# One core, attention into two mixer MLPs: the last two attention heads and the first MLP weights are placed anew

## The reference

```python
# attention: q, k, v are [2, 8, 768, 64]: 16 heads of 768 tokens
q_bucket, k_bucket = hash bits of q @ proj, k @ proj
scores = 64 ** -0.5 * (q @ k.T), -1e9 where q_bucket != k_bucket
attn = exp(scores - rowmax) / (rowsum + 1e-9);  x = attn @ v          # -> [2, 768, 512]
# first MLP
u = x + real(fft over tokens and features of x)
x = u + relu(layernorm(u) @ w_ch1) @ w_ch2
# second MLP
h = gelu(x @ w_in); a, v = h[..., :512], h[..., 512:]
x = x + (a * (w_sg @ (layernorm(v) * g_ln) + b_sg)) @ w_out
```

## Time and profile before

| | |
|---|---|
| median of 3 runs | 727.71 us (727.67 to 727.96) |
| the profiled execution | 727.84 us, of which the span of instructions is 726.0 us |
| PE busy | 713.9 us (98%) |
| DVE busy | 480.6 us (66%) |
| ACT busy | 382.2 us (53%) |
| POOL busy | 347.7 us (48%) |
| chain that ended last | PE 88%, DVE 7%, all else under 2% each |
| granted TensorE clock | full in all 40 slices |

### The profile page before, as it was taken

The page is one execution under the profiler, slowest core; times in us unless marked ns, Lnnn a source line. Parts: engine busy times, 40 slices in busy tenths (PEclk is TensorE's granted clock), DMA queues, the critical chain, the costliest instruction groups (busy, mean ns, idle before and its releaser), DMA issues.

```text
span 726.0 us, 11758 instructions
## 1 busy us (share of the span) xinstructions
PE 713.9 (98%) x3905; PEld 589.8 (81%) x3905; DVE 480.6 (66%) x701; ACT 382.2 (53%) x708; POOL 347.7 (48%) x341
## 2 busy tenths in 40 slices
PE   9999999999999999999999999999999999999998
PEld 8856666666675899988888888999998888888886
DVE  6877778787876799885655578544434675347533
ACT  4777888788876535554444554445442454125300
POOL 4178878887887920044633142546642355005400
PEclk9999999999999999999999999999999999999999
DMA  4332323232323150032211211822003000010001
GB/s 96 69 77 62 83 56 76 61 81 55 76 65 109 54 175 1 1 97 78 58 59 59 59 58 33 287 81 65 30 1 145 1 1 1 29 59 1 0 15 73
DMA packets 71076, 45.20 MB, mean 62 GB/s; under 512 B 44996, under 2 KB 61560, under 8 KB 70520
## 3 DMA queue, kind: packets, MB, share of 16 engines
q1 hardware_dynamic: 70456, 41.19, 20.7%
q0 software_dynamic: 576, 3.43, 1.3%
HBM read 35.42 MB, written 3.15 MB: 53 GB/s over the span
## 4 chain that ended last, share of the span: by engine, by line
PE 88%; DVE 7%; issue 1%; ACT 1%; POOL 1%; DMA 1%; SPq 0%; POOLq 0%; ACTq 0%; DVEq 0%
PE PS L814 83%; DVE un L2018 2%; DVE mneg L1780 1%; PE PS L838 1%; PE PS L1101 1%; PE PS L1318 1%; PE PS L1272 1%; DMA ops<-mrow 1%; PE PS L1263 1%; PE PS L953 1%; DVE st L2006 0%; DVE W1L L2051 0%; DVE ops L1751 0%; DVE ops L1772 0%; DVE ops L1745 0%
## 5 line engine op out<-in xcount | busy, mean ns | idle before, releaser
L814 PE MATMUL PS<-ops 98*128 98x384 f32 (+1 forms) x576 | 134.8, 359 | 3.4 <-DMA ops<-mrow 1.1
L814 PEld LDWEIGHTS PS<-ops 98*128 98x128 f32 (+1 forms) x576 | 95.4, 190 | 44.1 <-ACT E L1387 19.6
L1780 DVE TENSOR_REDUCE mneg<-PS 128x1 f32<-128x768 f32 x96 | 91.5, 956 | 36.9 <-PE PS L814 36.2
L1387 ACT ACTIVATE E<-PS 128x384 f32<-128x384 f32 x192 | 83.5, 487 | 44.7 <-PE PS L814 43.9
L664 POOL TENSOR_TENSOR esum<-esum,E 128x768 f32<-128x768 f32 x56 | 102.5, 1830 | 2.8 <-ACT E L1387 0.3
L649 POOL TENSOR_TENSOR W2L<-W2R,W2H 128x1024 fp32r<-128x1024 f32 x16 | 38.8, 2426 | 111.8 <-ACT W2H L1371 111.8
L2067 DVE SCALAR_TENSOR_TENSOR hL<-pre,hH 128x384 fp32r<-128x384 f32 x42 | 43.8, 1043 | 51.1 <-ACT hH L1632 51.1
L814 PE MATMUL PS<-BH,W1H 128*128 128x384 f32 x228 | 76.9, 337 | 0.4 <-DVE hL L2067 0.2
L814 PE MATMUL PS<-BH,W1L 128*128 128x384 f32 x228 | 76.9, 337 | 0.0
L814 PE MATMUL PS<-BL,W1H 128*128 128x384 f32 x228 | 76.2, 334 | 0.0
L814 PE MATMUL PS<-W2H,hH 128*128 128x512 f32 x192 | 75.5, 393 | 0.0
(11 more groups left out here) (211 smaller groups left out, 1595.1 us busy)
## 6 DMA issues: line engine op xcount, KB each, us to landing
W1R<-in_moe_w_ch_dram SPq DMA_DIRECT2D x32, 256.0 KB, 3.1
W2R<-in_moe_w_ch_dram SPq DMA_DIRECT2D x32, 256.0 KB, 2.9
ops<-ops SPq DMA_DIRECT2D x30, 192.0 KB, 3.0
qk<-in_k_dram SPq DMA_DIRECT2D x32, 96.0 KB, 2.4
qk<-in_q_dram SPq DMA_DIRECT2D x32, 96.0 KB, 2.4
vn<-in_v_dram SPq DMA_DIRECT2D x32, 96.0 KB, 2.4
out_dram<-X SPq DMA_DIRECT2D x12, 256.0 KB, 2.0
WsgR<-in_moe_w_sg_dram SPq DMA_DIRECT2D x1, 2304.0 KB, 8.1
```

The costliest lines, as they stand in the source:

```text
L814: return pe.matmul(dst, lhs, rhs, start=start, stop=stop, **kw)
L1387: act.activation(A["E"][:, e_slot(t, 0, kt), half(a)], PS[:, ST_BANK + a, 0:HALF], ACT.Exp, scale=EXP_SCALE).then_inc(exp_done, 1)
L1780: dve.tensor_reduce(A["mneg"][:, s, j:j + 1], PS[:, bank:bank + 2, 0:HALF], AX.XY, ALU.max, negate=True).then_inc(max_done, 1)
```

## The change

- `late` now holds for head 15 alone; head 14 takes the ordinary form. So POOL gets five `sum_exponentials` for it at time 14, ACT `raw_output` and `raw_sums` at time 15, PE `denominators` and `turn_back`, SP `place_sums`. The separate output bank of head 15 is given up.
- PE's time 15 is written out as `last_head`: scores and values of head 15 alternate by key tile, with head 14's last values and `denominators` ahead of `scores(2)`, and its `turn_back` ahead of `scores(4)`. Head 15's last values, once at time 16, are part of it.
- ACT: `weights_hi(0)` and `w2_upper(0)` leave time 14 and come behind `fold_hi` of passes 2 and 3.
- POOL: `weight_sums(1)` moves from time 14 to time 15; `first_weights_lower` and `w2_lower(0)` come behind the attention, each ahead of a `reciprocal_deviation` of the layer norm; T1L is loaded at time 14, between the fourth and the fifth sum; T2H and T2L are loaded at the end of time 15.
- DVE: `fold_lo(0)` goes ahead of head 14's `head_output`.

```diff
         def late(t, ahead):
-            return not t.looped and t.head(ahead) >= HEADS - 2
+            return not t.looped and t.head(ahead) >= HEADS - 1
...
@@ POOL
-                if not t.looped and t.head(0) == HEADS - 1:
-                    pool.wait_ge(rows_in, 32 * (HEADS - 1))
-                    load_first_table(A["T1L"], t1_lo)
-                    load_second_tables()
...
                 if t.has(1):
                     matches(t, 1)
+                if not t.looped and t.head(0) == HEADS - 2:
+                    pool.wait_ge(rows_in, 32 * (HEADS - 1))
+                    load_first_table(A["T1L"], t1_lo)
                 if t.has(0) and not late(t, 0):
                     sum_exponentials(t, 0, 4)
-                if not t.looped and t.head(0) == HEADS - 2:
+                if is_last(t):
                     weight_sums(1)
-                    first_weights_lower()
-                    w2_lower(0)
                 if t.has(-1):
                     finish_head(t, -1)
+                if is_last(t):
+                    load_second_tables()
...
-            for block in range(2):
-                reciprocal_deviation(0, block)
+            first_weights_lower()
+            reciprocal_deviation(0, 0)
+            w2_lower(0)
+            reciprocal_deviation(0, 1)
@@ PE
+            def last_values(t, kt):
+                g, s = t.head(0), t.slot(0)
+                if kt == 0:
+                    pe.wait_ge(v_in[s], 32 * t.turn(0) + 32)
+                    pe.wait_ge(mean_done, g + MEAN_FREE)
+                    pe.wait_ge(vsum_step, g + 1)
+                    mm(PS[:, PV_BANK, MEAN_AT:MEAN_AT + D], ones[:, :], A["vsum"][:, s, :], True, True)
+                pe.wait_ge(exp_done, 2 * T * g + 2 * kt + 2 + EXP_FREE)
+                for j in range(T):
+                    last = mm(PS[:, PV_BANK, j * (D + 1):(j + 1) * (D + 1)], A["E"][:, e_slot(t, 0, kt), tile(j)],
+                              A["vn"][:, s, kt, :], False, kt == T - 1, skip_group_check=True)
+                if kt % 2:
+                    last.then_inc(pv_step, 1)
+
+            def last_head(t):
+                scores(t, 0, 0)
+                scores(t, 0, 1)
+                values(t, -1, 2)
+                denominators(t, -1)
+                scores(t, 0, 2)
+                last_values(t, 0)
+                scores(t, 0, 3)
+                last_values(t, 1)
+                turn_back(t, -1)
+                scores(t, 0, 4)
+                last_values(t, 2)
+                scores(t, 0, 5)
+                for kt in range(TH, T):
+                    last_values(t, kt)
@@ ACT
                 if t.has(-1) and not late(t, -1):
                     raw_output(t, -1)
+                if is_last(t):
+                    raw_sums(t, -1)
...
-                if t.has(-1) and not late(t, -1):
+                if t.has(-1) and not late(t, -1) and not is_last(t):
                     raw_sums(t, -1)
...
-                if not t.looped and t.head(0) == HEADS - 2:
-                    weights_hi(0)
...
-                if not t.looped and t.head(0) == HEADS - 2:
-                    w2_upper(0)
...
                 if b + 1 < B:
                     fold_hi(2 * b + 2)
                     fold_hi(2 * b + 3)
+                    weights_hi(0)
+                    w2_upper(0)
@@ DVE
+                if pass1:
+                    fold_lo(0)
                 if t.has(-1):
                     head_output(t)
                 if pass1:
-                    fold_lo(0)
                     fold_features(1, 0)
```

More of the change, by code:

```diff
@@ L261, in late, with is_last @@
         def late(t, ahead):
-            return not t.looped and t.head(ahead) >= HEADS - 2
-        def out_bank(t, ahead):
-            return SUM_BANK if late(t, ahead) and t.head(ahead) == HEADS - 1 else PV_BANK
+            return not t.looped and t.head(ahead) >= HEADS - 1
+        def is_last(t):
+            return not t.looped and t.head(0) == HEADS - 1
         def e_sum(t, ahead):
@@ L918, in values @@
             def values(t, ahead, part):
-                g, s, bank = t.head(ahead), t.slot(ahead), out_bank(t, ahead)
+                g, s, bank = t.head(ahead), t.slot(ahead), PV_BANK
                 if part == 0:
                     pe.wait_ge(v_in[s], 32 * t.turn(ahead) + 32)
[L922 to L925, removed]
+                    pe.wait_ge(mean_done, g + MEAN_FREE)
                     pe.wait_ge(vsum_step, g + 1)
@@ L929, in values @@
                 for kt in (2 * part, 2 * part + 1):
[L930 to L937, removed]
-                last.then_inc(pv_step, 1)
+                    for a in range(2):
+                        last = mm(PS[a * D:(a + 1) * D, bank, 0:HALF], A["vn"][:, s, kt, 0:D],
+                                  A["E"][:, e_slot(t, ahead, kt), half(a)], kt == 0, kt == T - 1)
+                last.then_inc(pv_step, 1)
+            def last_values(t, kt):
+                g, s = t.head(0), t.slot(0)
+                if kt == 0:
+                    pe.wait_ge(v_in[s], 32 * t.turn(0) + 32)
+                    pe.wait_ge(mean_done, g + MEAN_FREE)
+                    pe.wait_ge(vsum_step, g + 1)
[21 more added lines that the diff above has]
+                    last_values(t, kt)
             def denominators(t, ahead):
@@ L1049, in one_time @@
                 t = Time(it, u)
+                if is_last(t):
+                    last_head(t)
+                    return
                 if t.has(0):
@@ L1057, in one_time @@
                     scores(t, 0, 1)
-                if t.has(-1):
+                if t.has(-1) and not late(t, -1):
                     values(t, -1, 2)
@@ L1795, in value_mean @@
                 dve.wait_ge(x_done, g - 1 + X_FREE)
-                dve.tensor_scalar(A["vmean"][:, t.slot(-1, 2), :], PS[:, out_bank(t, -1), MEAN_AT:MEAN_AT + D], 1.0 / S, None,
+                dve.tensor_scalar(A["vmean"][:, t.slot(-1, 2), :], PS[:, PV_BANK, MEAN_AT:MEAN_AT + D], 1.0 / S, None,
                                   ALU.mult).then_inc(mean_done, 1)
@@ L1803, in head_output @@
                     dve.wait_ge(pv_step, PV_PARTS * g + PV_PARTS)
-                    bank, at = out_bank(t, -1), MEAN_AT + D
+                    bank, at = PV_BANK, MEAN_AT + D
                     raw = PS[:, bank, 0:T * (D + 1)].rearrange("p (j w) -> p j w", j=T)
```

## The result

| | before | after |
|---|---|---|
| median | 727.73 us (727.67 to 727.96) | 740.82 us (740.58 to 741.41) |
| profiled execution | 727.84 us, span 726.0 | 740.58 us, span 738.7 |
| granted TensorE clock, mean over the span | full | 0.982 |

The ratio is 1.0182 (interval 1.0169 to 1.0196): 13.1 us slower, where 3.0 were forecast. The sign and the place were right, the size was four times too small.

The account below looks back on a forecast made before the run. PE was taken as the bound, with DVE nearly full in the first transform. 727.84 (profiled run) + 2.7 (attention) + 0.3 (moved weights) = 730.84, median 0.13 lower: 730.7 us; own range 729.3 to 731.9, range with rivals 726.8 to 733.2.

Parts of the forecast that it names:

- What bounds the kernel: Whole span: PE busy for 98%; in the first transform, 263.0 to 282.0, DVE is nearly full too, 17.63 of 19.0 us.
- What PE saves: Head 14's three parts of values in ordinary form save 3.6 us, denominators and turn_back add 1.25: net 2.4 us less.
- the first limit: scores(15, 0) waits for head 15's row maxima, placed by SP: starts at 244.0, gain 1.4 us, wait 1.0 us.
- The second limit: denominators(14) waits for POOL's fifth sum, which takes turns with DVE's folds: PE waits 2.9 us, bounds 0 to 2.9.
- the bound of 249.9: On POOL at time 14: the fifth sum's end if POOL wins the first turn, against 250.4 as walked.
- rival C: DVE's fold_tokens(1) gets ahead of the fifth sum: PE waits 4.7 us, total 732.5 us; chance 0.12.
- PE and DVE from there: After denominators(14): head 15's values end at 263.4, second_transform(0) gets DVE's result at 275.35; term +2.7 us, bounds -1.8 and +4.5.
- The forecast without the clock: Whole kernel: the walk's total with no clock fall counted, 730.7 us.
- the term for the moved weights: After the attention: W1's lower halves and w2_lower(0) on POOL meet DVE's work; +0.3 us, bounds 0 and 1.2.
- rival D: PE's waits of 1.0 and 2.9 us cost its clock: 4.5 us of work at half speed add about 2.3, 733.0 us; chance 0.08.
- Rival A: POOL at 239 to 247.5: turns are loose, PE's saving comes through, -1.8 us, 725.9 us; chance 0.14.

Follow-up runs that it names:

- alt_early_output: Kernel before with head 15's scores and values alternating, and on DVE its mean and output read ahead of two folds: 728.06 us, ratio 1.0003.
- alt_weights: Kernel before with the weights moved as in the change and head 15 alternating, head 14 still in late form: 729.03 us, ratio 1.0018.
- short_sums: Changed kernel with sums 2 to 5 of head 14 on POOL cut to 8 of 768 columns: 728.51 us, ratio 0.9998.
- fill: Changed kernel with nine float32 identity matmuls, results never read, put on PE ahead of denominators(14): 732.44 us, ratio 1.0059.
- wide_short: Changed kernel with 12 matmuls of 384 columns, results never read, behind scores(15, 2): 734.0 us, ratio 1.0088.
- fill_both: Changed kernel with nine identity matmuls ahead of denominators(14) and eight more ahead of second_transform(0): 731.47, 734.46, 739.59 and 742.12 us, ratio 1.0102.
- weights_only: Kernel before with only the weights moved as in the change, heads 14 and 15 late and in old order: 728.84 us, ratio 1.0008.
- stall_attention: Kernel before with one added PE wait for a tiny DMA ahead of values(14, 2): 741.6, 742.9 and 744.5 us, ratio 1.0216.
- wide_after_fall: Changed kernel with 24 matmuls of 384 columns, results never read, behind scores(15, 2): 735.0 us, ratio 1.0096.
- stall_mlp: Kernel before with the added PE wait for a tiny DMA in the first MLP, step 6: four runs 729.54 to 729.86, two 733.0 and 733.3 us; ratio 1.0039.

## Why the prediction was wrong

**What bounds the kernel: right.** PE first, DVE nearly full from 263 us on. Three kernels that ended the attention 1.5 to 3.2 us earlier (alt_early_output, alt_weights, short_sums) all met DVE there.

**What PE saves, and the first limit: right.** 1.44 us per part, `scores(15, 0)` 1.3 us earlier in the profile (with the earlier start of that trace taken off), where 1.4 were walked, and a wait of 0.92 where 1.0 was walked.

**The second limit: right in mechanism and nearly in size.** The wait was 2.27 us where 2.9 were walked. The second sum won the first turn (issued at 238.67, Z at 238.69), which the walk had as the bound of 249.9; one of the two small POOL operations came between Y and Y, the other ran beside the last Y, and the fifth sum ended at 250.0 on the time scale of the trace before, instead of 250.4. The order of fifth sum and `fold_tokens(1)` was the walked one, so rival C did not come. What the turns did not give is the fold's length of 4.00 us, with its end at 252.3. It should have had its turn after the fifth sum, at 249.7; instead POOL's next operation, which began 1.4 us after the fold and ran its usual 1.00 us from 249.67, went ahead of it too, in fill and wide_short as well. What the Trainium skill says of the shared port (SBUF — State Buffer, "Who interferes with whom"), that the engine which issues second waits for the whole instruction, fits the fold and the fifth sum, issued 0.4 us earlier; it does not fit this next operation.

**PE and DVE from there: right at full clock, in part by luck.** The transform starts at 263.5 in fill (263.35 in its own trace), walked 263.4. But two errors cancel in this: the first matmul of head 15's values comes at 252.8 instead of 252.2, since the fold was held longer, and from there PE needs 10.7 us instead of 11.2. PE's wait for DVE is 2.2 us, walked 2.15. The forecast without the clock was 730.7; the runs of this order at full clock took 731.40 (fill) and 731.47 (fill_both). Of the missing 0.7 us, 0.3 to 0.4 are in the term for the moved weights (0.3 taken, 0.6 to 0.7 in wide_short and weights_only), and 0.2 in the start of `second_transform(0)` (275.6 on the scale of before, walked 275.35).

**The clock: this is the step that failed.** The forecast's sum has no term for it; it stood in rival D with 0.08 and +2.3 us. Two things in it were mis-sized. *The price*: I took the length of a fall from the start of the kernel, 4.5 us. There PE does `keep_clock` matmuls and wide ones; behind the wait of this change it does late-form values of 65 columns. Measured: 27.3 us low. From the first matmul of head 15's values to the transform PE takes 20.16 us (252.53 to 272.69) where fill takes 10.67, so 9.5 more, and to the end of the first transform 12.0 more; 2.2 of this is taken back, as the wait for DVE vanishes beside a slower PE. That leaves 9.8 at `second_transform(0)` (285.06 against 275.42, each from its own start of the values), and 9.4 between the times, 740.82 less 731.40 at full clock. *The chance*: the fall came in four of four runs of the change, and with an added wait of 1.75 us in the three runs of stall_attention (means of 0.977 to 0.982 in both). I had argued that no wait of the trace before was long enough to show it, and made this a reason for a small chance; it was a reason for a wide one. With the measured 9.4 in place of 2.3 the forecast's 730.7 becomes 740.1; that is a check of the sum, and no derivation of the price.

The Trainium skill's rule, that an idle array is put to half its clock until it has been busy again (TensorE: Matmul & The Clock Gate, "What's actually happening"), pointed at the right mechanism. The runs show more than it: in the change, stall_attention and the low run of fill_both, PE was busy without a break in the windows from 256 to 268 and stayed at half speed; the clock came back at 278.3, 279.0 and 277.6, 4 to 7 us after the first matmuls of 194 columns. With matmuls of 384 columns right behind the wait it fell for a few microseconds at most (wide_short, wide_after_fall), and with 384 and 512 columns it fell briefly or not at all (stall_mlp).

**Rival A** (the saving comes through) would have failed even with loose turns: short_sums had no collision at all and came out level with before. `second_transform(0)` starts 1.0 us earlier there and not 1.8 (271.72 in its own trace, against 272.82), the moved weights take some 0.7 back, and a fall of 3.4 us behind PE's wait for DVE takes up to 1.7 (half of it) more. The bound left out the last.

Left open: which of column count, number format and share of time spent loading weights makes the clock stay low under the late-form matmuls. They differ from the wide ones in all three, and no run separates them. Nor is it settled what decides whether the clock falls at all: behind the same wait it fell in the change and not in the profiled run of wide_short, and in the same stretch it fell for long in two runs of four of fill_both and in none of five of fill.

## What to carry to other kernels

A wait of 2 us on a TensorE-bound stretch was priced here by what stood behind it: before wide dense matmuls it cost its own length (at times 3.4 us more), before small ones 14 to 17 us. So when a change puts a join of two engines in PE's path, find the last producer's neighbours on the shared port first, and look at the form of the matmuls behind it; if they are small, the possible fall of the clock is the largest term of the sum, not a remark. And before paying for an earlier end of one stage, check that the engine which bounds the next stage can start earlier too: here DVE could not.

## What the runs showed of the hardware

- Behind a PE wait of 1.75 or 2.27 us with float32 matmuls of 65 columns and scores after it, the granted clock was half for 27.3 us (stall_attention and the change), in the change with PE busy for all of the windows from 256 to 276. With 12 or 24 matmuls of 384 columns put behind the same wait, no run had a mean clock under 0.995, and in the profiled one with 12 it never fell.
- The fall came 1.2 us behind the wait in the change, before the first small matmul, and 2.1 us behind it in stall_attention. At one later place a wait of 2.2 to 2.3 us was followed by a low stretch of 3.4 us in each of three profiles (fill, short_sums, alt_weights), with matmuls of 256 columns behind it.
- Colliding operations of DVE and POOL, both reading two operands from SBUF, ran in turns at lengths of 0.9 and 1.8 us: three sums in 6.84 us and two Z in 5.14 us over the same 7 us. The turns are not strict: a fold of 1.75 us, begun 0.4 us after a sum, took 4.00 us, as POOL's next operation went ahead of it as well.
- Three DVE `tensor_scalar` tiles from SBUF to SBUF took 3.27 us instead of 1.45 where POOL's W2L of 2.39 us began 0.3 us before them.
